# A long convolution and two expert stages on one core: the inverse transform's groups as a loop instead of written out

## What is computed

```python
def _attn_ref(x, v, pos_emb, w1, w2):
    h_filt = (np.maximum(pos_emb @ w1, 0.0) @ w2) * np.exp(-0.01 * pos)[:, None]
    Uf = np.fft.rfft(x * v, n=2 * S, axis=1)
    Hf = np.fft.rfft(h_filt, n=2 * S, axis=0)
    y = np.fft.irfft(Uf * Hf[None, :, :], n=2 * S, axis=1)[:, :S, :]
    return x * y

def _moe_ref(x, modality_id, w_gate, modality_bias, w1, w2):
    logits = x @ w_gate + modality_bias[modality_id]
    e_idx = np.argmax(logits, axis=1)
    probs = softmax(logits)
    gate_w = probs[np.arange(N), e_idx]
    for e in range(E):
        mask = e_idx == e
        out[mask] = gate_w[mask, None] * (np.maximum(x[mask] @ w1[e], 0.0) @ w2[e])
    return out
```

## Time and profile before

| | |
|---|---|
| Device time, median of 3 runs | 2397.1 us |
| Lowest and highest | 2391.37 and 2403.07 us |
| The profiled execution: time, span | 2405.55 us, 2403.3 us |
| TensorE busy (matmuls) | 1995.1 us, 83% |
| VectorE, ScalarE, GpSimd busy | 1359.6 us (57%), 998.3 us (42%), 775.4 us (32%) |
| q8, instruction loads, whole span | 37 packets, 0.61 MB |

### The profile page before, as it was taken

How to read it: one execution, slowest core, us unless ns; L and a number is a source line. 1 busy time by engine, 2 the same in 40 slices (tenths; PEclk the granted TensorE clock), 3 DMA queues, 4 the chain that set the end, 5 groups by cost and what they waited for, 6 DMA issues and landing times. The chain is left out here.

```text
span 2403.3 us, 35753 instructions
## 1 busy us (share of the span) xinstructions
PE 1995.1 (83%) x9744; PEld 1639.1 (68%) x9744; DVE 1359.6 (57%) x3564; ACT 998.3 (42%) x2175; POOL 775.4 (32%) x738
## 2 busy tenths in 40 slices
PE   6577878686657675199999999999679999999996
PEld 4474567454647564178888887888558888888885
DVE  2397859774435353256666665666535555555552
ACT  3363333232222121045455554545335555555553
POOL 2143215330344555403232322222403333333333
PEclk9689998897667766599999999999889999999998
DMA  6657866786645563355555555555256666666662
GB/s 203 179 150 255 270 181 170 221 279 204 206 156 197 184 227 120 139 191 192 205 190 205 189 203 188 188 207 179 92 191 225 223 221 224 219 220 224 223 219 79
DMA packets 164823, 471.11 MB, mean 196 GB/s; under 512 B 24634, under 2 KB 80750, under 8 KB 135113
## 3 DMA queue, kind: packets, MB, share of 16 engines
q1 hardware_dynamic: 129416, 385.43, 49.0%
q0 software_dynamic: 24064, 61.17, 7.5%
q10 hardware_dynamic: 11264, 23.57, 3.2%
HBM read 365.29 MB, written 109.49 MB: 198 GB/s over the span
## 5 line engine op out<-in xcount | busy, mean ns | idle before, releaser
L1151 DVE SCALAR_TENSOR_TENSOR m_hid<-m_pH,m_hid 128x512 fp32r<-128x512 f32 x832 | 574.5, 691 | 406.5 <-ACT m_hid L1105 330.3
L1105 ACT ACTIVATE m_hid<-m_pH 128x512 fp32r<-128x512 f32 x832 | 501.0, 603 | 614.4 <-PE m_pH L1033 585.4
L1223 POOL DMA_INDIRECT rows<-m_rows,m_idx x208 | 204.0, 981 | 522.9 <-DVEq L1190 464.0
L1031 PE MATMUL m_pH<-m_xT,m_w 128*128 128x512 f32 x832 | 353.2, 425 | 11.4 <-DVE m_hid L1151 5.1
L1227 POOL DMA_INDIRECT out_dram<-m_rows,m_token x208 | 203.9, 980 | 434.2 <-ACT m_rows L1119 384.5
L1033 PE MATMUL m_pH<-m_xT,m_w 128*128 128x512 f32 x832 | 327.1, 393 | 0.0
L1032 PE MATMUL m_pH<-m_xT,m_w 128*128 128x512 f32 x832 | 326.9, 393 | 0.0
L1044 PE MATMUL m_pO<-m_hid,m_w 128*128 128x512 f32 x832 | 326.4, 392 | 0.0
L1046 PE MATMUL m_pO<-m_hid,m_w 128*128 128x512 f32 x832 | 326.0, 392 | 0.0
L1045 PE MATMUL m_pO<-m_hid,m_w 128*128 128x512 f32 x832 | 324.1, 390 | 0.0
L927 POOL DMA_INDIRECT rows<-oi_rows,oi_idx x192 | 194.3, 1012 | 226.7 <-ACT oi_raw_logits L880 129.2
(11 more groups left out here) (154 smaller groups left out, 2669.7 us busy)
## 6 DMA issues: line engine op xcount, KB each, us to landing
m_w<-halves_w SPq DMA_DIRECT2D x104, 1024.0 KB, 5.0
m_w<-halves_next_w SPq DMA_DIRECT2D x104, 1024.0 KB, 5.1
m_x<-rows SPq DMA_DIRECT2D x104, 264.0 KB, 4.3
pr_mats<-in_inner_dram SPq DMA_DIRECT2D x92, 256.0 KB, 3.9
inner_back<-pr_c SPq DMA_DIRECT2D x92, 256.0 KB, 3.5
oi_C<-inner_back SPq DMA_DIRECT2D x32, 728.0 KB
halves_w<-pr_parts POOLq DMA_DIRECT2D x16, 1024.0 KB
halves_next_w<-oi_parts ACTq DMA_DIRECT2D x32, 512.0 KB
```

What stands on the lines that cost most here:

```text
L1031: nc.tensor.matmul(out, high, xT[:, s % 2, 0], start=True, stop=False)
L1105: nc.scalar.activation(hid[:, s % 2, c, 0], pH[:, c % 2], ACT.Relu).then_inc(H_high, 1)
L1151: nc.vector.scalar_tensor_tensor(hid[:, s % 2, c, 1], pH[:, c % 2], 0.0, hid[:, s % 2, c, 0].bitcast(F32), ALU.max, ALU.subtract).then_inc ...
L1223: pool.indirect_dma_start(next_rows, bass.IndirectOffsetOnAxis(r.idx[:, s, t:t + 1], 0), rows[:, s, t, :], None, bounds_check=E * CAP + TI ...
```

## The change

```diff
+        def nth(s, turn):
+            return turn * 2 + s // 2
...
+        def own(ap, i):
+            return ap[:, bass.ds(i, 1), :].rearrange("p a n -> p (a n)")
...
-            for i in range(GROUPS):
-                s = i % 2
-                if i >= 2:
-                    sp.wait_ge(Y_ready, 2 * (i - 1))
+            def load(i, s, turn):
+                sp.wait_ge(Y_ready, i * 2 + 2)
...
+                    sp.dma_start(C[:, s % 2, half].rearrange("k e t w -> k e (t w)"),
+                                 src[bass.ds(i, 1), 0:KR].rearrange("a k e w -> (a k) e w")).then_inc(C_in[s % 2], 16)
...
+            pipeline(sp, GROUPS, 4, [(load, 0)])
...
         def _(pe):
+            pe.sem_inc(Y_ready, 4)
+            pe.sem_inc(G_ready, 2 * CC)
...
-                if i >= 1:
-                    pe.wait_ge(odd_copied, 2 * (i - 1) + half + 1)
-                    pe.wait_ge(y_done, 2 * (2 * (i - 1) + half + 1))
+                pe.wait_ge(odd_copied, i * 2 + (half + 1))
+                pe.wait_ge(y_done, i * 4 + (2 * half + 2))
...
-            for i in range(GROUPS + 2):
-                if i >= 2:
-                    sums(i - 2)
-                if i < GROUPS:
-                    outer(i, 0)
-                if 1 <= i <= GROUPS:
-                    gate(i - 1)
-                if i < GROUPS:
-                    outer(i, 1)
+            pipeline(pe, GROUPS, 4, [(sums, 2), (halved(outer, 0), 0), (gate, 1), (halved(outer, 1), 0)])
...
         def _(dve):
+            dve.sem_inc(y_done, 4)
+            dve.sem_inc(x1_done, 4)
+            dve.sem_inc(L_read, 2)
+            dve.sem_inc(P_read, 1)
+            dve.sem_inc(w_low, 2)
...
-                c.after(nc.vector.tensor_copy(rows[:, i % 4, :, TOKEN].bitcast(U32), numbers[:, i]))
+                c.after(nc.vector.tensor_copy(rows[:, s, :, TOKEN].bitcast(U32), own(numbers[:, :, :], i)))
...
+            pipeline(dve, GROUPS, 4, [(put, 2), (halved(mix, 0), 0), (choose, 1), (halved(mix, 1), 0), (low, 0)])
...
-                                         pG[:, cc % 2, 128:128 + B * E], ACT.Copy).then_inc(G_read, 2)
+                                         pG[:, cc % 2, 128:128 + B * E], ACT.Copy).then_inc(G_read, 1)
...
+            pipeline(act, GROUPS, 4, [(halved(copy_odd, 0), 0), (copy_back, 1), (exp, 1), (halved(copy_odd, 1), 0),
+                                      (high, 0), (store, 1)])
...
+            pool.sem_inc(rows_free, 4)
...
-            for i in range(GROUPS + 1):
-                if i < GROUPS:
-                    scatter(i)
-                if i >= 1:
-                    settle(i - 1)
+            pipeline(pool, GROUPS, 4, [(scatter, 0), (settle, 1)])
```

More of the change, by code:

```diff
@@ L697, in inverse_stage, with halved @@
         w_high, w_low = sem("w_high"), sem("w_low")
+        def nth(s, turn):
+            return turn * 2 + s // 2
+        def halved(step, half):
+            return lambda i, s, turn: step(i, s, turn, half)
+        def own(ap, i):
+            return ap[:, bass.ds(i, 1), :].rearrange("p a n -> p (a n)")
         block = ctx.enter_context(nc.Block())
@@ L728, in _, with outer @@
             pe.wait_ge(gates_made, 2)
-            def outer(i, half):
+            def outer(i, s, turn, half):
                 if half == 0:
-                    pe.wait_ge(C_in[i % 2], 32 * (i // 2 + 1))
-                if i >= 1:
-                    pe.wait_ge(odd_copied, 2 * (i - 1) + half + 1)
-                    pe.wait_ge(y_done, 2 * (2 * (i - 1) + half + 1))
+                    pe.wait_ge(C_in[s % 2], nth(s, turn) * 32 + 32)
+                pe.wait_ge(odd_copied, i * 2 + (half + 1))
+                pe.wait_ge(y_done, i * 4 + (2 * half + 2))
                 for eo in range(2):
@@ L775, in _, with mix @@
         @block.vector
         def _(dve):
[L777 to L780, removed]
+            dve.sem_inc(y_done, 4)
[3 more added lines that the diff above has]
+            dve.sem_inc(w_low, 2)
+            def mix(i, s, turn, half):
+                dve.wait_ge(odd_copied, i * 2 + (half + 3))
+                dve.wait_ge(x1_done, i * 2 + (half + 3))
@@ L790, in mix, with choose @@
+                dve.wait_ge(G_ready, i * CC + CC)
+                nc.vector.tensor_tensor(x1T[:, s % 2, half], y[:, half].rearrange("p m c -> p (m c)"),
+                                        xT[:, s % 2, half].rearrange("p m c -> p (m c)"), ALU.mult
                                         ).then_inc(x1_done, 1)
-            def choose(i):
+            def choose(i, s, turn):
                 c = Chain(dve, chain_l, i, 4)
                 for m in range(2):
-                    c.after(nc.vector.tensor_tensor(biased[:, m], r.spread(is_mod[:, m, i], n),
+                    c.after(nc.vector.tensor_tensor(biased[:, m], r.spread(own(is_mod[:, m], i), n),
@@ L847, in _ @@
         def _(act):
+            act.sem_inc(odd_copied, 2)
+            act.sem_inc(G_read, 2)
+            for s in range(2):
+                act.sem_inc(w_out[s], 32)
             r.load(act, w_gate, route_d)
@@ L895, in store @@
                 for layer in range(2):
                     dst = halves_d[layer].rearrange("e p h (a f) -> e p h a f", a=2)
[L897 to L910, removed]
+                    act.dma_start(dst[bass.ds(nth(s, turn), 1), :, :, s % 2].rearrange("e p h f -> p (e h) f"),
+                                  parts[:, s % 2, :, layer].bitcast(F32)).then_inc(w_out[s % 2], 16)
```

131 lines of the change are left out of this document (52 added, 79 removed).

## The result

| | Before | Changed |
|---|---|---|
| Median, 16 runs each | 2404.09 us | 2417.05 us |
| Lowest to highest | 2372.29 to 2427.79 | 2404.02 to 2432.19 |
| Ratio, 95% interval | | 1.010 (1.0065 to 1.0135) |
| Profiled execution, span | 2403.3 us | 2405.0 us |
| Stage: first instruction to end of last scatter | 577.98 to 1000.19, 422.2 us | 572.32 to 1004.86, 432.5 us |

What follows compares the result with a forecast made beforehand. The stage was taken to be bound by TensorE's signals coming late while GpSimd scatters. Register instructions 3 plus back edges 3 gave 6 us: 2411.6 against the profiled execution, 2403 us against the median shown; own range 2391 to 2415, all cases 2364 to 2434.

Steps and rivals of the forecast that it cites:

- What bounds the stage: Sixteen-group stage, 23.2 us a group: TensorE's signals come late while GpSimd scatters, from 4 to 5 us into a run until it ends.
- A single, 21.0 us a group: Pattern in the stage: TensorE signal, one group's scatter run, next signal only when that run is over; 21.0 us a group.
- double: Pattern in the stage: the signal slips through mid-run, two groups' scatters run back to back, 51.4 us for two groups.
- Waits, totals, the head's increments (0): Waits and semaphore totals unchanged; extra increments at the stage's head hidden by a 19.8 us DMA wait: 0, uncovered under 1 us.
- SyncE (0): SyncE's loads with register addresses: late by 0.1 to 0.3 us at most, wanted a whole group later, so 0.
- scatters (0): GpSimd's scatters in the stage: the same 192, each 0.98 us long in the looped stage as here, so 0.
- Register instructions (3 us; bound 18): About 15 on the signal-to-scatter path, 0 to 1.5 us a group; 0.25 taken for twelve looped groups, 3 us.
- stretched path: Rival, 18%: register instructions between signal and scatter cost 18 us instead of 3, plus back edges: 2420, up to 2436.
- Back edges (3 us): Loop jumps in the stage, three passes, priced from ScalarE's 1.6 us a pass in the expert loop: up to 4.8, 3 taken.
- the long body doesn't stay: Rival, 7%: each back edge jumps to absent code and waits about 3 us for loading; up to 12 us, 2415.
- Instruction loading was the stall: Rival, 10%: TensorE stops lagging from the ninth group on, GpSimd's 16.0 us a group sets the beat: 2345.
- singles: Rival, 15%: slower gating on TensorE tips doubles into singles, each pair saving 9.4 us, three in the looped part: 2375.

## Why the prediction was right and where it failed

- *What bounds the stage*: right for the chips of the late kind, and for the loop too: "remote" 173.9 us, lags in all passes. They set in somewhat earlier than the 4 to 5 us I gave: matmuls that ended 3.9 us into a run (groups 6, 10 and 14) were signalled 7.5 us late. I hadn't thought that another chip might not show it. It was alike for all kernels profiled in one set of runs and differed between sets; each chip was used once, so chip and time of measuring aren't told apart.
- *A single, 21.0 us a group*: misread. The last of the five groups from 822.60 to 927.36 us is the first half of a double; the four before it took 22.2 us each from scatter run to scatter run (830.03 to 918.69). A pair of singles saves 7 us against a double, not 9.4. The number of doubles is five in both profiles, so it doesn't explain the 10.3 us.
- *Waits, totals, the head's increments (0)*: right. The first outer matmul still waits 19.2 us for the gates' DMA (19.8 before); with 128 more increments at VectorE's head it waits 20.0. My price without that cover was too low: these increments started 0.09 us apart, so twenty are 1.9 us, not under 1.
- *SyncE (0), scatters (0)*: nothing in the traces speaks against it.
- *Register instructions (3 us; bound 18)*: 0. Copy to scatter is 7.5 us inside a pass against 7.4, at most 1.2 us over the twelve groups. The rival "stretched path" falls.
- *Back edges (3 us)*: **this is the term that failed.** Measured 8.4 and 8.2 us, 16.6 in all, on VectorE, on the path, for code that had to be loaded. I priced them from an expert loop whose body of 249 instructions stays. The stage lost less than the sum of the gaps in the first pair of profiles (10.3 us). Counted between the first scatters of groups, 4 to 6 and 8 to 10, where the gaps lie, took 51.5 and 51.9 us instead of 45.4 and 43.9, 14.2 us more; the rest took 3.8 less. The late start also changes where the doubles fall: 10 to 12 is one now and took 5.6 us more, 12 to 14 no longer is and took 7.3 less.
- *The rival "the long body doesn't stay" (7%)*: the right mechanism with nearly the right price (12 us), on the wrong engine. I asked it of TensorE alone, whose body stayed (queue q8 loaded no block between 752 us and the end of the stage), though the listing had 280 instructions on VectorE, more than the expert loop's 249. (Counted in the trace, TensorE's bodies have 789 and, in the expert loop, 619 instructions, not 784 and 571; nothing hangs on it.) What the Trainium skill (Runtime: NRT & Kernel Launch, Instruction fetch mechanics) says of a taken branch to absent code is what VectorE shows: 5.1 us, and 3.3 for the next block. The same section of the Trainium skill gives other engines than TensorE 32 KiB, 512 instructions, which are four blocks of 8 KB; a body that touched four was not kept. It gives blocks of 16 KiB for every engine, which q8 has here (12 blocks, 0.20 MB) but q14 has not (3 blocks, 0.02 MB): the measured sizes decide. Its remark of two blocks, by which TensorE's body would not fit, isn't borne out: 789 instructions are more than three blocks of 256, and they stayed.
- *Forecast 2403, 1.0025 times the median shown*: measured 1.010, and 1.013 on the other chip of the late kind. I gave slower 35%, no change 38%. With the one question asked of VectorE too, slower would have been the likeliest case. That the time fell into the wide range is owed to its width, not to the sum: the sum has 3 us for the back edges where 16.6 were measured, and 3 for register instructions where about none were.
- *Instruction loading was the stall, singles*: both fell; lags and doubles are there in the loop.

## What to carry to other kernels

Before writing a program as a loop, count for every engine how many instruction blocks its body touches, not only how long it is, and which engine's back edge lies on the path; twenty idle instructions ahead of the loop were worth 1.2% here (2402.9 against 2432.8 us). A gain or loss that one chip shows may be hidden on another that has a different bound: compare only on one chip, and ask of each row which of the two it comes from. Where one engine issues long runs of indirect DMAs and another's signals come late, try short pauses, and measure them on both kinds of chip.

## What the runs showed of the hardware that was new

- In three of the five sets of runs TensorE's signals come up to 24 us late while GpSimd issues indirect DMAs, in the other two hardly; to the kernel before that is 103 to 112 us (2399 to 2404 against 2292 to 2296). The kernel before was profiled on the first chip only; on the others, that it is of the same kind as the kernels beside it is taken from its time. The cause wasn't found. Two pauses in a group's scatters (3.6 us from one scatter's start to the next instead of 1.3) reduced the lateness to 6.4 us at most.
- A loop body of 280 instructions stays on VectorE where it touches three 8 KB blocks and doesn't where it touches four, at 8.3 us a back edge; one of 216 that begins at nearly the same place but touches three stays.
- These pauses cost GpSimd 4.7 us a group (twice 3.62 - 1.29), 20.9 us between groups' first scatters on average, and still gave 0.6%.
